# Second layer in five unequal blocks of tokens, with activations split in place

## The reference

```python
def _moe_ref(x, w_gate, w_val, w_out):          # 512 -> 1536 -> 512
    g = x @ w_gate
    silu = g * (1.0 / (1.0 + np.exp(-g)))
    val = x @ w_val
    return (silu * val @ w_out).astype(np.float32)

def _moe2_ref(x, w_in, w_out, alpha):           # 512 -> 2048 -> 512
    h = x @ w_in
    g = np.maximum(h, 0.0) + alpha * np.minimum(h, 0.0)
    return (g @ w_out).astype(np.float32)
```

## Time and profile before

| | |
|---|---|
| median of 3 runs | 950.58 us (950.41 to 951.32) |
| the profiled execution | 951.09 us, of which the profile's span is 949.0 us |
| PE busy | 931.3 us, 98% of the span, 7944 matmuls |
| DVE busy | 504.5 us, 53% |
| ACT busy | 279.3 us, 29% |
| POOL busy | 140.2 us, 15% |
| granted clock of TensorE | 1.00, its upper level (2.4 GHz), throughout |

### The profile page before, as it was taken

The page is one execution under the profiler, slowest core; times in us unless marked ns, Lnnn a source line. Parts: engine busy times, 40 slices in busy tenths (PEclk is TensorE's granted clock), DMA queues, the critical chain, the costliest instruction groups (busy, mean ns, idle before and its releaser), DMA issues.

```text
span 949.0 us, 19252 instructions
## 1 busy us (share of the span) xinstructions
PE 931.3 (98%) x7944; PEld 857.6 (90%) x7944; DVE 504.5 (53%) x996; ACT 279.3 (29%) x707; POOL 140.2 (15%) x167
## 2 busy tenths in 40 slices
PE   4999999999999999999999999999999999999998
PEld 3899999999988888898999999999999999999997
DVE  8899777544466665454323344444444444444443
ACT  5665444322233433223223422111111111111111
POOL 7876110000011000000025620000000000000000
PEclk9999999999999999999999999999999999999999
DMA  9763323211122221200053320020100200100000
GB/s 278 237 210 97 105 82 109 78 50 41 41 83 77 76 75 62 86 22 14 4 169 123 111 93 0 1 67 1 42 25 1 67 1 1 67 1 1 34 1 34
DMA packets 31077, 63.24 MB, mean 67 GB/s; under 512 B 3344, under 2 KB 13584, under 8 KB 30992
## 3 DMA queue, kind: packets, MB, share of 16 engines
q1 hardware_dynamic: 30992, 62.02, 20.5%
HBM read 52.57 MB, written 9.44 MB: 65 GB/s over the span
## 4 chain that ended last, share of the span: by engine, by line
PE 90%; DVE 4%; issue 2%; ACT 1%; DMA 1%; SPq 1%; POOL 0%; DVEq 0%; ACTq 0%
PE ps L1090 50%; PE ps L1135 21%; PE ps L1118 14%; PE ps L1038 1%; PE ps L974 1%; DMA vsrc_early<-vsrc 1%; PE ps L984 1%; PE ps L1051 1%; PE ps L1022 1%; DVE v_d_one L768 1%; DVE row_padded L805 1%; DVE gated L922 0%; DVE h_lo L912 0%; DVE neg_max L796 0%; SPq L365 0%
## 5 line engine op out<-in xcount | busy, mean ns | idle before, releaser
L672 ACT CAST h_hi<-hidden 128x384 fp32r<-128x384 f32 (+3 forms) x168 | 86.3, 513 | 419.6 <-DVE hidden L945 329.4
L1090 PE MATMUL ps<-x_hi,w_hi 128*128 128x416 f32 (+2 forms) x573 | 199.1, 347 | 0.0
L1090 PE MATMUL ps<-x_lo,w_hi 128*128 128x416 f32 (+2 forms) x573 | 193.1, 337 | 0.0
L1090 PE MATMUL ps<-x_hi,w_lo 128*128 128x416 f32 (+2 forms) x573 | 193.1, 337 | 0.0
L912 DVE TENSOR_TENSOR h_lo<-hidden,h_hi 128x384 fp32r<-128x384 f32 (+3 forms) x168 | 106.4, 633 | 72.2 <-ACT h_hi L672 72.2
L943 DVE TENSOR_SCALAR gated<-ps,alpha_sb 128x384 f32<-128x384 f32 x96 | 59.3, 618 | 158.5 <-PE ps L1090 158.5
L1135 PE MATMUL ps<-w_hi,h_hi 128*128 128x512 f32 x288 | 112.3, 390 | 0.5 <-DVE h_lo L912 0.5
L1135 PE MATMUL ps<-w_hi,h_lo 128*128 128x512 f32 x288 | 112.6, 391 | 0.0
L1090 PEld LDWEIGHTS ps<-x_hi,w_hi 128*128 128x128 f32 x573 | 107.6, 188 | 5.5 <-DVE gated L922 0.3
L1135 PE MATMUL ps<-w_lo,h_hi 128*128 128x512 f32 x288 | 112.4, 390 | 0.0
L1090 PEld LDWEIGHTS ps<-x_hi,w_lo 128*128 128x128 f32 x573 | 107.7, 188 | 3.3
(11 more groups left out here) (140 smaller groups left out, 1470.7 us busy)
## 6 DMA issues: line engine op xcount, KB each, us to landing
w_home<-w SPq DMA_DIRECT2D x68, 256.0 KB, 3.9
qk<-qk SPq DMA_DIRECT2D x30, 436.0 KB, 3.7
vsrc_one<-vsrc SPq DMA_DIRECT2D x58, 144.0 KB
vwin<-vwin SPq DMA_DIRECT2D x30, 192.0 KB, 2.4
x_raw<-y_t SPq DMA_DIRECT2D x6, 768.0 KB, 5.8
out<-y_sb SPq DMA_DIRECT2D x5, 768.0 KB, 4.0
y_t<-y_sb SPq DMA_DIRECT2D x2, 896.0 KB, 4.7
y_t<-y_sb SPq DMA_DIRECT2D x2, 832.0 KB, 4.4
```

What stands on the lines that cost most here:

```text
L672: nc.scalar.copy(h_hi[r][:, 0:width], hidden[r][:, 0:width]).then_inc(h_hi_ready, 1)
L1090: mm = nc.tensor.matmul(out_ps, w[:, piece, 128 * k:128 * k + 128], x_parts[low][:, k, :], start=(k == 0 and n == 0), stop=(k == KC - 1 an ...
```

## The change

The second layer's six blocks of 384 tokens become four of 512 and one of 256 (`SPANS2`). A block of 512 tokens holds four banks for its outputs, so the banks are dealt out in five sets. The low part of an activation is written over `hidden`: `hidden0` and `hidden1` are given the addresses of `h_lo0` and `h_lo1`, and DVE therefore waits for `h_used` before it writes `hidden`, in both layers. The widest tiles (`h_hi`, `h_lo`, `gated`, `y_sb`, `x_raw`, `x2_*`) grow to 512 columns. In the last block the input product of chunk 15 stands ahead of the output product of chunk 13. The last bank is copied and stored in two halves of 256 columns, by DVE. SP's loop over the blocks is written out.

```diff
-TB2 = 384
-NB2 = TOKENS // TB2
+SPANS2 = (512, 512, 512, 512, 256)
+NB2 = len(SPANS2)
+TB2 = SPANS2[0]
+TILES2 = [span // 128 for span in SPANS2]
...
+LAST_PARTS = (slice(0, DM // 2), slice(DM // 2, DM))
...
-        y2_ps = [[bank(m) for m in banks] for banks in ((6, 7, 2), (0, 1, 3))]
+        y2_ps = [[bank(m) for m in banks] for banks in ((6, 7, 2, 3), (0, 1, 6, 7), (2, 3, 0, 1), (6, 7, 2, 3), (0, 1))]
...
+        with ExitStack() as unsplit_h:
+            hidden = [sb(f"hidden{r}", [128, WIDEST], where=unsplit_h) for r in range(2)]
         h_lo = [sb(f"h_lo{r}", [128, WIDEST], F32R) for r in range(2)]
...
-                for cols in (slice(0, DM // 2), slice(DM // 2, DM)):
-                    nc.vector.tensor_copy(y2_sb[:, 2, cols], banks[2][:, cols]).then_inc(y13_copied, 1)
+                for m in (1, 3):
+                    nc.vector.tensor_copy(y2_sb[:, m, :], banks[m]).then_inc(y13_copied, 1)
...
                     dve.wait_ge(gated_ready, s + 2)
+                    dve.wait_ge(h_used, s + 1)
+                    nc.vector.scalar_tensor_tensor(out=hidden[r][:, 0:span], in0=pre_ps[j][r], scalar=0.0, in1=gated[:, 0:span],
...
-            nc.vector.tensor_copy(y2_sb[:, 1, :], y2_ps[1][1]).then_inc(last_copied[1], 1)
+            for cols in LAST_PARTS:
+                nc.vector.tensor_copy(y2_sb[:, 1, cols], y2_ps[-1][1][:, cols]).then_inc(last_copied[1], 1)
...
-                    if c == 0 and m == 2:
-                        pe.wait_ge(y02_copied, 2 * j + 2 * NL1 + 4)
-                        pe.wait_ge(y13_copied, 2 * j + 2 * NL1 + 4)
+                    if c == 0 and m == 2:
+                        pe.wait_ge(y02_copied, 2 * j + 2 * NL1 + 3)
+                        pe.wait_ge(y13_copied, 2 * j + 2 * NL1 + 3)
...
+                    if j < NB2 - 1 or c < C2 - 1:
+                        inputs(c)
+                    if j == NB2 - 1 and c == C2 - 2:
+                        inputs(c + 1)
```

More of the change, by code:

```diff
@@ L141, in build @@
         gate_ps, val_ps = [bank(4)[:, 0:span] for span in SPANS], [bank(5)[:, 0:span] for span in SPANS]
-        pre_ps = (bank(4)[:, 0:TB2], bank(5)[:, 0:TB2])
-        y2_ps = [[bank(m) for m in banks] for banks in ((6, 7, 2), (0, 1, 3))]
+        pre_ps = [[bank(n)[:, 0:span] for n in (4, 5)] for span in SPANS2]
+        y2_ps = [[bank(m) for m in banks] for banks in ((6, 7, 2, 3), (0, 1, 6, 7), (2, 3, 0, 1), (6, 7, 2, 3), (0, 1))]
         first_banks = ((4, 5), (0, 1), (2, 3), (6, 7))
@@ L218, in build @@
         gated = sb("gated", [128, WIDEST])
-        hidden = [sb(f"hidden{r}", [128, WIDEST]) for r in range(2)]
         y_sb = sb("y_sb", [128, KC * WIDEST])
@@ L403, in load_x @@
             def load_x(j):
-                sp.dma_start(x_raw[:, :, :], y_t[:, :, bass.ds(TB2 * j, TB2)].rearrange("k p s -> p k s")).then_inc(x_in, 16)
+                span = SPANS2[j]
+                sp.dma_start(x_raw[:, :, 0:span], y_t[:, :, TB2 * j:TB2 * j + span].rearrange("k p s -> p k s")).then_inc(x_in, 16)
             def store_y(j):
@@ L413, in store_y2 @@
                 sp.wait_ge(y13_copied, 2 * j + 2 * NL1 + 6)
-                sp.dma_start(out[bass.ds(TB2 * j, TB2), :].rearrange("(t p) f -> p t f", p=128), y2_sb).then_inc(y_stored, 16)
+                sp.dma_start(out[TB2 * j:TB2 * j + TB2, :].rearrange("(t p) f -> p t f", p=128), y2_sb).then_inc(y_stored, 16)
             def load_pieces(first, end):
@@ L464, in _ @@
             load_x(1)
-            with sp.Fori(0, NB2 - 2) as j:
+            for j in range(NB2 - 2):
                 store_y2(j)
@@ L469, in _ @@
             store_y2(NB2 - 2)
[L471 to L474, removed]
+            sp.wait_ge(last_copied[0], 1)
+            sp.dma_start(out[TOKENS - 256:TOKENS - 128, :], y2_sb[:, 0, :]).then_inc(y_stored, 16)
+            for n, cols in enumerate(LAST_PARTS):
+                sp.wait_ge(last_copied[1], n + 1)
+                sp.dma_start(out[TOKENS - 128:TOKENS, cols], y2_sb[:, 1, cols]).then_inc(y_stored, 16)
+            sp.wait_ge(y_stored, 16 * (ALL + 1 + len(LAST_PARTS)))
         @block.gpsimd
@@ L660, in copy_out2 @@
                 act.wait_ge(y_stored, 16 * j + 16)
-                for m in (0, 1):
+                for m in (0, 2):
                     nc.scalar.copy(y2_sb[:, m, :], banks[m]).then_inc(y02_copied, 1)
@@ L689, in split_loaded_x_hi @@
                 act.wait_ge(x_in, 16 * j + 16)
-                nc.scalar.copy(x2_hi[half][:, k, :], x_raw[:, k, :]).then_inc(x_hi_ready, 1)
+                nc.scalar.copy(x2_hi[half][:, k, 0:SPANS2[j]], x_raw[:, k, 0:SPANS2[j]]).then_inc(x_hi_ready, 1)
             def first_block(j):
@@ L723, in second_block @@
                     if c == 0 and j:
-                        copy_out2(j + NL1 - 1, s, y2_ps[1 - half])
+                        copy_out2(j + NL1 - 1, s, y2_ps[j - 1])
                     elif c == 0:
@@ L732, in _ @@
             act.wait_ge(y_stored, 16 * ALL)
-            for m in (0, 2):
-                act.wait_ge(bank_ready, m + 1)
-                nc.scalar.copy(y2_sb[:, m, :], y2_ps[1][m]).then_inc(last_copied[m], 1)
+            act.wait_ge(bank_ready, 1)
+            nc.scalar.copy(y2_sb[:, 0, :], y2_ps[-1][0]).then_inc(last_copied[0], 1)
         @block.vector
@@ L942, in second_block @@
                     dve.wait_ge(pre_ready, s + 1)
-                    nc.vector.tensor_scalar(gated[:, 0:TB2], pre_ps[r], 0.0, alpha_sb[:, c:c + 1], ALU.min, ALU.mult).then_inc(gated_ready, 1)
+                    nc.vector.tensor_scalar(gated[:, 0:span], pre_ps[j][r], 0.0, alpha_sb[:, c:c + 1], ALU.min, ALU.mult).then_inc(gated_ready, 1)
                     dve.wait_ge(gated_ready, s + 2)
-                    nc.vector.scalar_tensor_tensor(out=hidden[r][:, 0:TB2], in0=pre_ps[r], scalar=0.0, in1=gated[:, 0:TB2],
+                    dve.wait_ge(h_used, s + 1)
+                    nc.vector.scalar_tensor_tensor(out=hidden[r][:, 0:span], in0=pre_ps[j][r], scalar=0.0, in1=gated[:, 0:span],
                                                    op0=ALU.max, op1=ALU.add).then_inc(hidden_ready, 1)
-                    low_part(s, r, TB2)
+                    low_part(s, r, span)
                     if c == 0 and j:
-                        copy_out2(j + NL1 - 1, s, y2_ps[1 - half])
+                        copy_out2(j + NL1 - 1, s, y2_ps[j - 1])
                     elif c == 0:
@@ L1129, in outputs2 @@
                 pe.wait_ge(h_lo_ready, s + 1)
-                for m in range(TT):
+                for m in range(TILES2[j]):
                     if c == 0 and m == 2:
-                        pe.wait_ge(y02_copied, 2 * j + 2 * NL1 + 4)
-                        pe.wait_ge(y13_copied, 2 * j + 2 * NL1 + 4)
+                        pe.wait_ge(y02_copied, 2 * j + 2 * NL1 + 3)
+                        pe.wait_ge(y13_copied, 2 * j + 2 * NL1 + 3)
                     for n, (w, low) in enumerate(PARTS):
@@ L1136, in outputs2 @@
                                               start=(c == 0 and n == 0), stop=(c == C2 - 1 and n == len(PARTS) - 1))
-                    if last_block and m < TT - 1:
+                    if last_block and m < TILES2[j] - 1:
                         mm.then_inc(bank_ready, 1)
@@ L1162, in second_block, with inputs @@
                 wait_for_x(j + NB + 1)
+                span = SPANS2[j]
+                x_here = (x2_hi[half][:, :, 0:span], x2_lo[half][:, :, 0:span])
+                def inputs(c):
+                    pe.wait_ge(hidden_ready, STEPS1 + C2 * j + c)
+                    pe.wait_ge(w_ready, P1 + 2 * c + 1)
+                    products(pre_ps[j][c % 2], 2 * c, x_here).then_inc(pre_ready, 1)
                 for c in range(C2):
                     s = STEPS1 + C2 * j + c
-                    pe.wait_ge(hidden_ready, s)
-                    pe.wait_ge(w_ready, P1 + 2 * c + 1)
-                    products(pre_ps[c % 2], 2 * c, (x2_hi[half], x2_lo[half])).then_inc(pre_ready, 1)
+                    if j < NB2 - 1 or c < C2 - 1:
+                        inputs(c)
+                    if j == NB2 - 1 and c == C2 - 2:
+                        inputs(c + 1)
                     if c or j:
-                        outputs2((c - 1) % C2, j if c else j - 1, s - 1, y2_ps[half if c else 1 - half])
+                        at = j if c else j - 1
+                        outputs2((c - 1) % C2, at, s - 1, y2_ps[at])
                     else:
```

8 lines of the change are left out of this document (4 added, 4 removed).

## The result

| | before | changed |
|---|---|---|
| median of 18 runs | 951.08 us (950.13 to 952.25) | 952.69 us (951.55 to 954.36) |
| ratio | | 1.0020, 95% interval 1.0014 to 1.0026 |
| span of the profiled execution | 949.0 us | 951.4 us |
| first input matmul of the second layer to the last output matmul, starts | 545.83 to 945.38 = 399.5 us | 546.47 to 947.81 = 401.3 us |

The kernel became 0.2% slower where 0.22% faster was forecast. Ahead of that layer the runs scatter: over the kernels of this study its first matmul started anywhere from 544.7 to 547.7 us.

A forecast was written before the change was run, and what follows sets the result against it. The second layer was taken as a PE-bound matmul stream, priced from start to start. 951.09 - 1.7 (input products) - 0.3 (end) - 0.1 (last bank) = 949.0 us, or 948.5 on the medians' scale; range 947.2 to 950.8.

The forecast's parts named there:

- the signs that the prediction named as making it wrong: A matmul distance above 130 ns at 256 columns, or an early stretch longer by 0.5 us.
- Input products: Second layer: 1152 matmuls of 384 columns become 768 of 512 and 192 of 256; 199.7 to 198.0 us, gaining 1.7.
- the lower bound: Input products: 512-column matmuls with the smaller fixed part seen at 416 columns, 226.7 ns each, 1.0 us more gain.
- Output products: Second layer: 864 matmuls of 512 columns before and after, so no change in time.
- The rival "Tiles at new addresses slow some stretch": Moved tiles slow some stretch by 2 us or more: 952.5 us at least, slower; chance 4%.
- The floor at 256 columns: Rival on 256-column matmuls: 133 ns gives 951.1 us, no gain (5%); 188 ns gives 961.7, slower (4%).
- The chain: Per-chunk work between input and output product: grows from 2.5 to about 3.1 us, hidden behind 5.5 us of matmuls.
- the borders: Between blocks: larger bank copies, DVE's 1.4 us against 0.75 before, cost nothing.
- the loads: Block loads and stores of 1 MB instead of 768 KB hide in most of an 88 us block.
- DVE's further wait in the first layer: `hidden` waiting for `h_used`: forecast 0; rival 0.7 us over 12 early chunks, 949.2 us, chance 14%.
- The end: Stall before the last output product falls from 0.64 to 0.32 us, gaining 0.3; rival of no gain, 949.1 us, 12%.
- The last bank: Final copy and store in two halves: copy 0.17 us later, store 0.25 saved; 0.1 us gained, between +0.3 and -0.2.

The follow-up runs named there:

- the stream: Kernel before with PE-only matmul streams of several widths, all from w, added behind its last output product: 226.7 ns at 512 columns, 120.0 at 256.
- The two experiments: Changed kernel with the order at the end undone: layer 401.8 us, 954.6 whole; with the last chunk's `hidden` in its own tile: 400.9 us, 954.2 whole.
- streams without: Changed kernel with PE-only streams reading `x2`, w and `h` added behind its last output product: in turn, 2.763 and 2.770 us for 12 matmuls.

## Why the prediction was wrong, point by point

Forecast were 2.1 us less than before (1.7 + 0.3 + 0.1), measured are 1.6 more by the medians and 1.8 more in the layer. Two terms of the sum failed: the output products, put at nothing, cost 2.3 us more, and the input products gave 0.2 us in place of 1.7. Behind both stands one assumption, that a matmul has a fixed part over its streaming time that goes with it into other surroundings. None of the signs that the prediction named as making it wrong showed.

- **Input products, 1.7 us less forecast, 0.2 measured.** The failing step here is the price of 512 columns: "For 512 columns as moving operand I take the 228 ns of the output products". They cost 230.2. The 226.7 of the lower bound is what they cost at another address; that x2 as moving operand could cost more than w was not considered at all. The count (192 matmuls fewer) and the 256-column price were right: 118.2 ns against 119.3 forecast.
- **Output products, "Nothing", measured +2.3 us, the larger miss.** The number of matmuls is the same, but not their distance: 228.05 before, 230.8 now. The mean of 228 in the earlier trace rows already hid three matmuls at 229 to 233 ns behind each input product and six at 226.7 (means by place over 94 groups); I took the mean for a fixed part. What followed the input products was a price of the change from one kind of product to the other, and the change made it dearer (12 ns a chunk before, 50 after).
- **The rival "Tiles at new addresses slow some stretch"** had 4% and no row for it. It was near the cause, but the new addresses alone did nothing at 384 columns, and `x2` kept its place in 256 bytes (192 mod 256 before and after). The old place met a new width.
- **The floor at 256 columns** at 133 or 188 ns is not there: the distance is 118.2 ns in the changed kernel and 120.0 in the stream. The load rule of the Trainium skill ("TensorE: Matmul & The Clock Gate", section LDWEIGHTS; by it an estimate of 107 ns for 128 columns) lies below both, so these runs agree with it and don't test it. Unrounded, the rule's 128/1.2 and the streaming's 256/2.4 are the same 106.7 ns, so the prediction's "just fails to cover its load" was an effect of rounding.
- **The chain, the borders, the loads**: hidden, as forecast. PE waited for no engine inside the layer until its last output product.
- **DVE's further wait in the first layer** costs nothing. From the second `gated` to the eleventh the early stretch took 53.39 us before (38.54 to 91.93) and 53.35 after (39.65 to 93.00), and `hidden` still follows `gated` by 0.09 us (75.32 + 0.40 to 75.81). The first layer ended 0.6 us later than before, which lies inside the scatter of 3 us.
- **The end, 0.3 us**: right, 0.27 (a stall of 0.64 before and 0.38 now, against 0.32 forecast), and by the mechanism named. The two experiments show what the order gained, 0.46, and what the shared tile kept back, 0.43.
- **The last bank, 0.1 us**: from the last matmul's start to the end of the span 3.66 us before and 3.61 after, 0.06 by the unrounded times. With one execution each this can't be told from 0 or from 0.1.

## What to carry to other kernels

Price a matmul by the mean distance of its own group in its own surroundings, and then look inside the group: if single distances differ by 2 to 9 ns from the rest, or the same shape has lengths of 389 and 396 ns in one profile, the rest over the streaming time is not a fixed cost and can't be carried to another width. Change width and place of a streamed tile together: here the same edit was 0.2% slower than before with `x2` at 192 mod 256 and 0.4% faster at 128. A few unused bytes ahead of a tile are worth a run with each of the four places that are 64 bytes apart, at the final widths: the place that was best for 512 columns (128) was the worse of the two tried in the kernel with 384.

## What the runs showed of the hardware that I had not expected

- The start of the moving operand within 256 bytes, with the weights at 128, moves the distance of 512-column matmuls of rounded parts (float32r) between 226.7 and 233.3 ns, with DVE and ACT idle. With w as moving operand and every start at 128 mod 256 the distance of N columns, less N/2.4 ns, was 13.3 ns at 256, 320, 384 and 512 columns, but 15.0 at 416 and 16.0 at 448.
- A change from one kind of product to the other, or of width, can cost up to about 50 ns over the next ten matmuls, and depends on both sides. The outputs behind 384-column inputs cost 12 ns more with `x2` at 192 and 41 at 128; behind 512-column inputs 50 at 192, 17 at 0, and none at 128. The 41 ns came in the streams from w alone too. The pattern of 512 to 512 with `x2` at 192 was the same to a nanosecond in the kernel, with other engines at work, and in streams without.
- What produces this in the chip was not found, and stays open; so does why output matmuls that read only w and `h` carry a price set by the products ahead of them. Other pairs of places for weights and moving operand were not tried.
